# A chunked delta-rule attention with two MLPs: the first group's inverses taken on halves of 16, with the corners added by small matrix products, and the gate weights folded the other way round

## What is computed

```python
k_n = k / (np.linalg.norm(k, axis=-1, keepdims=True) + 1e-06)
for t in range(S):
    kt, vt, bt = (k_n[:, :, t], v[:, :, t], beta[:, :, t, None])
    y[:, :, t] = np.einsum('bhd,bhde->bhe', q[:, :, t], state)
    v_old = np.einsum('bhde,bhd->bhe', state, kt)
    state = state + bt[:, :, :, None] * np.einsum('bhd,bhe->bhde', kt, vt - v_old)
...
h = x @ w_in                       # then SoLU and layer norm -> ln
x = (ln * g_ln) @ w_out
...
logits = x @ w_gate                # argmax picks the expert
```

## Time and profile before

| | us |
|---|---|
| median of 3 runs | 424.25 (423.18 to 429.47) |
| the profiled execution | 423.3 |
| its span, first to last instruction | 421.6 |
| PE busy in the span | 388.5 (92%) |
| DVE busy | 304.7 (72%) |
| ACT busy | 226.2 (54%) |
| POOL busy | 66.9 (16%) |

### The profile page before, as it was taken

The page is one execution under the profiler, slowest core; times in us unless marked ns, Lnnn a source line. Parts: engine busy times, 40 slices in busy tenths (PEclk is TensorE's granted clock), DMA queues, the critical chain, the costliest instruction groups (busy, mean ns, idle before and its releaser), DMA issues.

```text
span 421.6 us, 13134 instructions
## 1 busy us (share of the span) xinstructions
PE 388.5 (92%) x5487; PEld 368.7 (87%) x5488; DVE 304.7 (72%) x596; ACT 226.2 (54%) x409; POOL 66.9 (16%) x80
## 2 busy tenths in 40 slices
PE   3887998979999999999998998999999999999991
PEld 3887897859989889999887998899999999999991
DVE  5899898796987778974257877768795694738650
ACT  2545643766441347652237844667775794629550
POOL 3100200000020000010030003404245144110211
PEclk9999999998999999999999996999999999999996
DMA  6997003960100183100139511263846648180000
GB/s 154 314 220 220 5 3 83 212 234 10 49 22 5 40 181 82 40 23 22 35 85 402 178 38 42 61 245 110 330 159 227 231 142 306 36 327 2 29 2 27
DMA packets 25574, 52.00 MB, mean 123 GB/s; under 512 B 4468, under 2 KB 19120, under 8 KB 25040
## 3 DMA queue, kind: packets, MB, share of 16 engines
q1 hardware_dynamic: 21216, 44.95, 34.0%
q0 software_dynamic: 3136, 4.73, 3.6%
q10 hardware_dynamic: 1168, 1.52, 1.7%
HBM read 44.30 MB, written 9.44 MB: 127 GB/s over the span
## 4 chain that ended last, share of the span: by engine, by line
PE 76%; DVE 15%; issue 4%; ACT 3%; POOL 0%; DVEq 0%; POOLq 0%; ACTq 0%
PE PS L573 11%; PE PS L575 11%; PE PS L574 10%; PE PS L1697 8%; PE PS L1551 4%; PE PS L1742 4%; PE PS L1752 4%; PE PS L1743 3%; PE PS L1603 3%; PE PS L1616 3%; PE PS L1709 2%; PE PS L1563 2%; PE PS L1577 2%; PE PS L1591 2%; PE PS L1470 2%
## 5 line engine op out<-in xcount | busy, mean ns | idle before, releaser
L573 PE MATMUL PS<-xTh,w1h 128*128 128x224 f32 (+3 forms) x198 | 56.1, 283 | 1.1 <-DVE hTl L482 0.5
L574 PE MATMUL PS<-xTl,w1h 128*128 128x224 f32 (+3 forms) x198 | 55.5, 280 | 0.0
L575 PE MATMUL PS<-xTh,w1l 128*128 128x224 f32 (+3 forms) x198 | 55.5, 280 | 0.0
L1697 PE MATMUL PS<-w_in_h,mlpT 128*128 128x512 f32 x144 | 46.3, 394 | 1.1 <-issue 1.1
L573 PE MATMUL PS<-w2h,hTh 128*128 128x384 f32 x136 | 46.1, 339 | 0.0
L575 PE MATMUL PS<-w2h,hTl 128*128 128x384 f32 x136 | 45.5, 335 | 0.0
L574 PE MATMUL PS<-w2l,hTh 128*128 128x384 f32 x136 | 45.5, 334 | 0.0
L482 DVE SCALAR_TENSOR_TENSOR hTl<-PS,hTh 128x384 fp32r<-128x384 f32 x64 | 35.3, 552 | 8.8 <-ACT hTh L378 5.3
L378 ACT ACTIVATE hTh<-PS 128x384 fp32r<-128x384 f32 x64 | 31.7, 495 | 15.9 <-PE PS L575 12.6
L573 PEld LDWEIGHTS PS<-xTh,w1h 128*128 128x128 f32 x198 | 37.9, 191 | 2.3 <-issue 1.1
L508 POOL DMA_INDIRECT out<-yo,oiu x24 | 24.3, 1012 | 89.7 <-ACT yo L389 81.7
(11 more groups left out here) (195 smaller groups left out, 905.1 us busy)
## 6 DMA issues: line engine op xcount, KB each, us to landing
w1r<-w SPq DMA_DIRECT2D x8, 1536.0 KB, 6.5
w2r<-w SPq DMA_DIRECT2D x8, 1536.0 KB
KP<-kv SPq DMA_DIRECT2D x3, 1536.0 KB, 11.4
out<-zero SPq DMA_DIRECT2D x12, 192.0 KB, 4.0
x<-rowst SPq DMA_DIRECT2D x12, 192.0 KB, 1.9
QT<-qt SPq DMA_DIRECT2D x5, 384.0 KB, 6.9
yx<-yx SPq DMA_DIRECT2D x12, 144.0 KB
XE<-w_out_t SPq DMA_DIRECT2D x1, 1536.0 KB, 6.4
```

Of the source, the lines that this page charges most:

```text
L573: pe.matmul(out_ap, lhs[0], rhs[0], start=first, stop=False)
L574: pe.matmul(out_ap, lhs[0], rhs[1], start=False, stop=False)
L575: return pe.matmul(out_ap, lhs[1], rhs[0], start=False, stop=final)
L1697: last = pe.matmul(PS[:, h_bank(g, n) + s, :], mlpT[:, n, x, c, :], w[:, c, o], start=(c == 0 and j == 0), stop=(c == KD - 1 and j == 2))
```

## The change

For group 0 alone the 32x32 blocks are inverted as two diagonal halves of 16 on VectorE (`lower_of_halves`, `fold_halves`, `rows_of_halves`, `place_halves`). The corner of each block, 16x16 below the diagonal, comes from two sets of products on TensorE: `crossing_products` multiplies the block of G by the factor of the first half, ScalarE copies the result with the sign turned and the upper half's rows set to zero (`crossing_part`), `factor_products` multiplies that by the factor of the second half, and VectorE adds it (`crossing_factor`), transposes the sum and copies its odd blocks (`rows_of_factor`). The gate folding is turned round: w_gate is stationary, the transposed w_out is streamed in 6 products of 512 columns, ScalarE copies the 8 rows, 8 transposes on TensorE turn them, and one VectorE instruction scales them. The loads of KT[1] are issued before everything that waits for the grams; the warm products become 4 and 5; VectorE's masking of the scores and the transpose of group 1 move ahead of the first solve; `solve(0, 0)` stands before `solve(0, 1)`.

```diff
+        HB = BL // 2
+        halves = Tm[:, 480:480 + BL * HB]
+        own_grams = St[:].rearrange("p s b a d -> p (s b a d)")[:, 0:NU * BL].rearrange("p (u j) -> p u j", j=BL)
+        crossing = QG[:, 0:NU * HB].rearrange("p (u j) -> p u j", j=HB)
...
+        def halves_at(b):
+            return PS[:, b, :].rearrange("p (u k) -> p u k", k=HB)
...
+                load_half(sp, KT[1], kt, 1, 0, ld_kt[1])
                 sp.wait_ge(kk, 4)
                 sp.dma_start(w_out_t_sb, w_out_t.rearrange("(c p) f -> p c f", p=P)).then_inc(ld_wt, 16)
...
                 sp.dma_start(w_raw[:, :, 0:DM], w_out.rearrange("(k p) n -> p k n", p=P)).then_inc(ld_wo, 16)
-                load_half(sp, KT[1], kt, 1, 0, ld_kt[1])
                 sp.dma_start(bet[1][:], beta[1]).then_inc(ld_bet[1], 16)
                 load_kv(0)
...
+                pool.memset(Tw[:, 0:BL * BL], 0.0).then_inc(t_clear, 1)
...
-                    pool.wait_ge(e_tb, g + 1)
+                    if g:
+                        pool.wait_ge(e_tb, g)
                     if g < 2:
                         pool.wait_ge(d_tb, g + 1)
...
-                strictly_lower(0)
+                strictly_lower_halves()
...
+                def keep_grams():
+
+                    act.wait_ge(e_as, 1)
+                    act.activation(own_grams, grams_at(0)[:, :, 0:BL], ACT.Copy).then_inc(e_gd, 1)
+
+                def crossing_part():
+
+                    act.wait_ge(q_cross, 4)
+                    act.wait_ge(lower_half, 1)
+                    act.activation(crossing, halves_at(0), ACT.Copy, scale=low_half[:, P // BL:P // BL + 1]).then_inc(e_cross, 1)
...
-                def fold():
+                def scale_w_out():
 
                     act.wait_ge(ld_wo, 32)
                     for k in range(KF):
                         last = act.activation(w_raw[:, k, 0:DM], w_raw[:, k, 0:DM], ACT.Copy, scale=gl[:, k:k + 1])
                     last.then_inc(wscaled, 1)
-                    act.wait_ge(wfold, 1)
-                    for k in range(KF):
-                        last = act.activation(w_raw[:, k, DM:RW], PS[:, 2, k * E:(k + 1) * E], ACT.Copy, scale=gl[:, k:k + 1])
-                    last.then_inc(wfolded, 1)
+
+                def take_gates():
+
+                    act.wait_ge(wfold, 2)
+                    act.activation(gate_rows, PS[0:E, 2:4, :].rearrange("p k n -> p (k n)"), ACT.Copy).then_inc(e_gates, 1)
+
+                def w_out_high():
+
                     act.wait_ge(wscaled, 1)
+                    act.activation(w_out_h[:, :, 0:DM], w_raw[:, :, 0:DM], ACT.Copy)
+
+                def w_gate_high():
+
                     act.wait_ge(wfolded, 1)
-                    act.activation(w_out_h[:], w_raw[:], ACT.Copy).then_inc(w_hi, 1)
+                    act.activation(w_out_h[:, :, DM:RW], w_raw[:, :, DM:RW], ACT.Copy).then_inc(w_hi, 1)
...
+                load_half(act, KT[1], kt, 1, 1, ld_kt[1])
                 odd_blocks(0)
                 roots(0)
+                keep_grams()
+                take_scores(0)
                 cross_blocks(0)
-                take_scores(0)
-                load_half(act, KT[1], kt, 1, 1, ld_kt[1])
-                fold()
                 odd_blocks(1)
-                lower_rows(0)
+                scale_w_out()
+                crossing_part()
+                take_gates()
+                roots(1)
+                cross_blocks(1)
+                w_out_high()
                 between(0)
                 lower_block(0)
-                roots(1)
-                cross_blocks(1)
+                w_gate_high()
...
+                def lower_of_halves():
+
+                    rows = halves.rearrange("p (r j) -> p r j", j=HB)
+                    dve.wait_ge(below, 1)
+                    link(dve.scalar_tensor_tensor(rows, rows, -1.0, gamT[:, :].unsqueeze(2).to_broadcast([P, BL, HB]), ALU.mult, ALU.mult))
+
+                def fold_halves(l):
+
+                    nb = HB // ST
+                    rows = halves.rearrange("p (r b l) -> p r b l", b=nb, l=ST)
+                    w = [P, HB, nb, l]
+                    t = Tm[:, 0:BL * nb * l].rearrange("p (r b m) -> p r b m", b=nb, m=l)
+                    for h in range(2):
+                        r = slice(h * HB, (h + 1) * HB)
+                        at = 480 + h * HB * HB
+                        of = Tm[:, at:at + nb * ST * (HB + 1)].rearrange("p (b s) -> p b s", s=ST * (HB + 1))
+                        last = dve.tensor_tensor(t[:, r], rows[:, r, :, l:l + 1].to_broadcast(w), of[:, :, l * HB:l * HB + l].unsqueeze(1).to_broadcast(w), ALU.mult)
+                    link(last)
+                    link(dve.tensor_tensor(rows[:, :, :, 0:l], rows[:, :, :, 0:l], t, ALU.add))
...
+                def rows_of_halves(b):
+
+                    j = ST * b
+                    n = HB - 1 - j
+                    both = halves.rearrange("p (h i j) -> p h i j", h=2, j=HB)
+                    w = [P, n, ST, j]
+                    t = Tm[:, 0:2 * n * ST * j].rearrange("p (r l k) -> p r l k", l=ST, k=j)
+                    for h in range(2):
+                        last = dve.tensor_tensor(t[:, h * n:(h + 1) * n], both[:, h, j + 1:HB, j:j + ST].unsqueeze(3).to_broadcast(w), both[:, h, j:j + ST, 0:j].unsqueeze(1).to_broadcast(w), ALU.mult)
+                    link(last)
+                    link(dve.tensor_tensor(t[:, :, 0:2], t[:, :, 0:2], t[:, :, 2:4], ALU.add))
+                    sums = Tm[:, 0:2 * n * ST * j].rearrange("p (h i l k) -> p h i l k", h=2, l=ST, k=j)
+                    for l in range(2):
+                        link(dve.tensor_tensor(both[:, :, j + 1:HB, 0:j], both[:, :, j + 1:HB, 0:j], sums[:, :, :, l], ALU.add))
+
+                def place_halves():
+
+                    both = halves.rearrange("p (h i j) -> p h i j", h=2, j=HB)
+                    to = Tw[:, :].rearrange("p (h s) -> p h s", h=2)[:, :, 0:HB * BL].rearrange("p h (i j) -> p h i j", j=BL)[:, :, :, 0:HB]
+                    dve.wait_ge(t_clear, 1)
+                    link(dve.tensor_tensor(to, both, gamT[:, :].rearrange("p (h j) -> p h j", h=2).unsqueeze(2).to_broadcast([P, 2, HB, HB]), ALU.mult))
+                    link(dve.tensor_copy(Tw[:, 0:BL * BL:BL + 1], gamT[:, :]))
+                    dve.transpose(T1u[:].rearrange("p u j -> p j u"), Ts.rearrange("p i j -> p j i")).then_inc(t_ready, 1)
+
+                def crossing_factor():
+
+                    dve.wait_ge(q_factor, 4)
+                    dve.tensor_tensor(T1u[:, :, 0:HB], T1u[:, :, 0:HB], halves_at(1), ALU.add).then_inc(d_factor, 1)
+
+                def rows_of_factor():
+
+                    dve.wait_ge(d_factor, 1)
+                    dve.transpose(TT64[:, :, 0], T1u[:]).then_inc(td_ready, 1)
+                    dve.wait_ge(td_ready, 2)
+                    for q in (3, 1):
+                        last = dve.tensor_copy(TT64[block(q), :, 1], TT64[block(q), :, 0])
+                    last.then_inc(d_tb, 1)
+
+                def gates_of_w_out():
+
+                    dve.wait_ge(gates_done, 1)
+                    dve.wait_ge(ld_wo, 32)
+                    dve.tensor_tensor(w_raw[:, :, DM:RW], PS[:, 2, 0:KF * E].rearrange("p (k e) -> p k e", e=E), gl[:, :].unsqueeze(2).to_broadcast([P, KF, E]), ALU.mult).then_inc(wfolded, 1)
...
-                    mask_first()
                     scales(1)
...
-                lower(0)
+                lower_of_halves()
                 for l in range(ST - 1, 0, -1):
-                    fold_steps(l)
-                for b in range(1, BL // ST):
-                    rows_of_t(b)
-                    if b == 6:
-                        dve.sem_inc(rows_near, 1)
-                place_factors(0)
+                    fold_halves(l)
+                for b in range(1, HB // ST):
+                    rows_of_halves(b)
+                place_halves()
                 place_rows(0)
-                lower_rows(0)
+                mask_first()
+                systems(1)
                 scale_v(0)
-                systems(1)
+                crossing_factor()
+                rows_of_factor()
                 lower_block(0)
+                gates_of_w_out()
...
-                def fold():
+                def fold(s, chunks):
 
                     pe.wait_ge(ld_wt, 32)
-                    pe.wait_ge(e_as, 1)
+                    pe.wait_ge(e_gd, 1)
                     pe.wait_ge(e_gx, 1)
+                    for c in chunks:
+                        last = pe.matmul(PS[0:E, 2 + s, :], wg[:, c, :], w_out_t_sb[:, c, s * 512:(s + 1) * 512], start=(c == 0), stop=(c == KD - 1))
+                    if c == KD - 1:
+                        last.then_inc(wfold, 1)
+
+                def turn_gates():
+
+                    pe.wait_ge(e_gates, 1)
                     for k in range(KF):
-                        for c in range(KD):
```

(48 more changed lines are left out.)

26 lines of the change are left out of this document (19 added, 7 removed).

## The result

The changed kernel takes 438.99 us (median of 4 runs, 438.33 to 440.82); the kernel before, run beside it, 426.63 (423.18 to 429.47). The ratio is 1.030 with a 95% interval of 1.020 to 1.040: slower by about 3%, where 421.8 us, a range up to 428.0 and "no change" were forecast. Spans of the two profiled executions: 436.4 us after, 421.6 before. The first solve, S, starts at 60.87 instead of 47.50, so 13.4 of the 14.8 us are lost ahead of S.

What follows compares the result with a forecast made beforehand. Dependent VectorE steps, then TensorE, were taken to bound the first solve's start. Moving it from 47.50 to 44.7 gains 2.8 us, less 0.3 for later VectorE work: 2.5 off, from the 424.25 median to 421.8 us; range 418.8 to 428.0.

Steps and rivals of the forecast that it cites:

- VectorE's part: Group 0's inversion on VectorE: 27 steps on halves take 9.8 us instead of 23.2, factor ready at 25.3 instead of 38.7.
- w_out and v were on time: Loads ahead of the first solve: w_out's scaling was to end at 30.6, v's at 35.3, hidden by 0.8 us.
- The price of a gate product at the lower level: TensorE's streamed gate products of 512 columns: 1.77 us each at the lower clock, 1.1 at the upper.
- The sets' own running time: Crossing and factor products on TensorE: 3.5 us a set, taken between 2.2 and 4.4.
- That S decides: Start of the first solve, 47.50 before, forecast 44.7: the span should move by what this start moves.
- The two sets of small products: Crossing and factor products on TensorE, 256 records each: priced from `between`'s 17.3 ns a record, 3.5 us a set taken.
- A: Rival: small products are cheap, 2.2 us a set; gain 3.7 us, up to 5, 419 to 420.6 us; chance 0.2.
- D: Rival: small-product sets are issue-bound, 7.4 us each; slower, 429 to 430 us; chance 0.07.
- TensorE: when it is free: TensorE before the crossing products: `grams(1)` ends at 20.4, four gate products at 27.0 with the clock rising at 26.4.
- Rival C: TensorE's clock stays at or falls to 1.2 GHz between 20 and 45 us: costs 5.6 us, 427.3 us; chance 0.13.

Runs made afterwards that it cites:

- the run with fillers: The changed kernel with two unread products of 64x384 zeros behind every 32 small products, three places in each set: 438.50 us, ratio 1.035 against the kernel before.
- the extra set: The kernel before with one unread set of 128 products of 32x32 weights and 16 columns behind `between`: ratio 1.018.
- the dense products: The kernel before with ten more dense 128-column warm products on zeros, unread, behind the first group's `between` products: ratio 1.011.

## Why the prediction was wrong

**Right.** VectorE's part, to 0.4 us: its factor was ready at 24.94 (forecast 25.3), 13.7 us earlier than before. w_out and v were on time: w_out's scaling ended at 34.5 and v's at 33.3, both ahead of what waits for them. The price of a gate product at the lower level was right (1.79 each at 39.58, forecast 1.77). The sets' own running time, 2.9 and 3.8 us for 3.5, was near, and that is partly luck: 3.5 was a choice between two rows, a set at the 9.8 ns a record of its first stretch would take 2.5, and the second set ran at the lower level. That S decides was right: 13.4 of 14.8 us.

**The step that failed** is "The two sets of small products". It priced them by the time of a record in `between`, 17.3 ns, and asked whether the array would be slower or faster. The array was faster than every row there was: 212 records in 2.07 us, 9.8 ns each. So rivals A and D were about a quantity that decides nothing; what D asks for, 7.4 us a set, came nearly true (6.4 and 4.9 us here, 6.7 alone) by another mechanism. The cost that the sum put at nothing is the loading of 512 instructions a set: 3.58 and 1.19 us of pauses in the sets, 4.61 and 1.41 ahead of them. The Trainium skill's 62 ns a matmul where hardware decode is off ("TensorE: Matmul & The Clock Gate", Part 1), an estimated 7.9 us a set, is not what happens either: 19.5 ns a product between pauses.

The same mechanism was missed in **"TensorE: when it is free"**: `grams(1)` was to end at 20.4 and ended at 28.3. The row of 3.69 us at 28 us was measured when its block had long arrived, behind 10.41 us of gate products with 48 records; moved ahead of them, it is the third set of 128 records in a row. S is 16.2 us later than the forecast of 44.7:

| term | us |
|---|---|
| four pauses for code (1.41 + 4.61 + 3.58 + 1.19), in the prediction nothing | +10.8 |
| lower clock: two gate products 1.4, warm products 0.9, `between` 1.4, `lower_block` to S 1.9 | +5.6 |
| QT landed later, behind the keys (scores from 11.90 instead of 10.74) | +1.2 |
| `grams(1)`, own running time 4.2 for 3.7 | +0.5 |
| first four gate products, 5.0 for 6.6 | -1.6 |
| the two sets, running time alone | -0.4 |

The sum is 16.1. **Rival C** named the clock, its place (20 to 45 us) and its price (5.6 us), and by its price 427.3; the clock term is indeed 5.6 us. That the sums agree is partly luck: C had 0.5 us for the first four gate products, which came out 1.6 shorter, and 1.5 for the way from `lower_block` to S, which lost 1.9. And it was thought of as something that gate products fail to raise. The clock did come up, at 31.1, and fell inside a pause that no part of the prediction had. How much of the 5.6 is a consequence of the pauses is shown in part: without them, in the run with fillers, the gate products (1.88), the warm products (1.16) and `between` (2.21) ran at the upper level, while `lower_block` (3.35) and the warm products behind it did not.

**What was there to be seen before.** The forecast ran from the first crossing product to the end of `lower_block` in 16 us (27.0 to 43). On that way stand 788 records, 6.2 blocks; at 3.7 us each they need 23 us with nothing else in the way, and 19 at the 3.1 us of the shortest block that ended in a pause (44.2 to 47.2 in the changed kernel). Counted from the forecast's 27.0, this estimate puts S at about 48 or later, where the kernel before has 47.5: the two sets in this place could not have brought it forward. In the kernel before, 272 records stand between 39.92 and 47.50, 2.1 blocks in 7.6 us or 3.6 us a block: it runs just at the pace at which code comes. The page of before has the instruction queue (43 packets, 0.70 MB, a share of 0.7%), and no term of the prediction is about it.

**Open.** What fills the 1.1 us ahead of a packet and the 1.4 us behind it in quiet. Why the clock fell at 53.8 in the run with fillers, with no pause over 0.7 us ahead of it, and at 45.6 in the kernel before with the turned gate products. And the 4 us by which spans behind S differ among versions whose code is the same there.

## What to carry to other kernels

Before work is turned into many small matmuls, count instructions as well as array time: in a straight program here 256 TensorE instructions, 128 f32 records, cost 3.1 to 3.9 us wherever they are used up faster than that and the DMA engines are quiet, and up to 10.8 where these are full. It pays to trade VectorE time for TensorE products only where TensorE's code arrives in time. Here a pause `<-issue` that came back every 128 records, with a packet of the instruction queue ending 1.2 to 1.7 us ahead of its end, was code and not the array; behind the longer ones the clock was at its lower level, a second cost.

## What was not expected of the hardware

- A block of code under load: from the start of the block at 16.14 to the next at 26.95, 10.8 us, with the DMA engines full (share 1.07); in quiet 3.1 to 3.9 where the block ended in a pause (44.2 to 47.2 in the changed kernel, 42.97 to 46.70 with the extra set, 43.1 to 47.0 with the dense products). The load delays the start of the packet, not the packet.
- An f32 32x32 product with 16 columns takes 19.5 ns when its code is there (two records of 9.8 ns), less than any row of the kernel before; at the lower level 29 ns (207 records in 2.96 us).
- The granted clock came up at 31.1 in the changed kernel, in the run of products with only 8 columns of weights and 512 streamed (28.20 to 33.2); in the kernel before, 48 records with 128 columns of weights and 8 streamed left it down.
- Within pauses of 3.58 and 2.49 us (at 38.0 and 45.9), and 1.6 us behind one of 3.30 us (at 40.8), the granted clock went to its lower level; in the run with fillers, with none over 0.7 us, it stayed up through both sets of small products and then fell at 53.8 all the same.
